# Moving the tail of one expert behind the head of the next in an eight-expert layer

## The reference, cut to what matters

```
disp[e, slot] = x[token]                       # up to 384 slots for each expert
h = np.maximum(np.einsum('ecd,edf->ecf', disp, w1), 0.0)    # 384 -> 1024
y = np.einsum('ecf,efd->ecd', h, w2)                        # 1024 -> 384
out[token] = gate_w[token] * y[expert_idx[token], pos[token]]
```

## Time and profile before

| | |
|---|---|
| median of 3 runs | 415.0 us (414.7 to 415.39) |
| the profiled execution, its own time | 415.56 us |
| its span, first to last instruction | 413.7 us |
| granted TensorE clock, mean | 0.997 |
| PE busy | 406.2 us, 98% |
| DVE, ACT, POOL busy | 242.4, 188.1, 231.4 us |
| chain of work that ended last | PE 88%, DVE 4%, issue 3%, DMA 3% |

### The profile page before, as it was taken

The page is one execution under the profiler, slowest core; times in us unless marked ns, Lnnn a source line. Parts: engine busy times, 40 slices in busy tenths (PEclk is TensorE's granted clock), DMA queues, the critical chain, the costliest instruction groups (busy, mean ns, idle before and its releaser), DMA issues.

```text
span 413.7 us, 9445 instructions
## 1 busy us (share of the span) xinstructions
PE 406.2 (98%) x3697; PEld 390.3 (94%) x3697; DVE 242.4 (59%) x576; ACT 188.1 (45%) x409; POOL 231.4 (56%) x239
## 2 busy tenths in 40 slices
PE   8999999999999999999999999999999999999995
PEld 8799799999999999999999999999999999999995
DVE  7787955376576547654663487785635546364522
ACT  4786553233333333333343455552645455474420
POOL 3789865567856685668234336065083562826531
PEclk9999999999999999999999999999999999999998
DMA  7998997214030403020018001827383845729000
GB/s 281 399 395 341 348 371 255 72 49 150 10 119 2 139 21 118 2 87 21 2 19 345 2 2 38 326 77 238 135 304 99 346 147 217 279 100 363 8 31 28
DMA packets 18650, 64.98 MB, mean 157 GB/s; under 512 B 2203, under 2 KB 11717, under 8 KB 16432
## 3 DMA queue, kind: packets, MB, share of 16 engines
q1 hardware_dynamic: 16672, 59.67, 39.5%
q0 software_dynamic: 1792, 4.73, 3.0%
q10 hardware_dynamic: 144, 0.00, 0.0%
HBM read 51.98 MB, written 13.21 MB: 158 GB/s over the span
## 4 chain that ended last, share of the span: by engine, by line
PE 88%; DVE 4%; issue 3%; DMA 3%; POOL 1%; ACT 1%; POOLq 0%; SPq 0%; DVEq 0%
PE bank L1369 26%; PE bank L1371 25%; PE bank L1370 24%; PE bank L1390 2%; DMA xrow<-slots 2%; PE bank L1419 1%; PE bank L1455 1%; PE bank L1459 1%; PE bank L1693 1%; PE bank L1448 1%; PE bank L1451 1%; PE bank L1546 1%; PE bank L1728 1%; PE bank L1729 1%; PE bank L1632 1%
## 5 line engine op out<-in xcount | busy, mean ns | idle before, releaser
L707 POOL TENSOR_TENSOR g_lo<-elu,g_hi 128x256 fp32r<-128x256 f32 x95 | 73.7, 777 | 86.9 <-ACT g_hi L882 86.6
L1369 PE MATMUL bank<-xt,wd_hi 128*128 128x256 f32 x285 | 80.5, 283 | 0.6 <-DVE elu L1197 0.6
L1371 PE MATMUL bank<-xt,wd_lo 128*128 128x256 f32 x285 | 80.4, 282 | 0.0
L1370 PE MATMUL bank<-xt,wd_hi 128*128 128x256 f32 x285 | 80.3, 282 | 0.0
L873 ACT ACTIVATE elu<-elu 128x256 f32<-128x256 f32 x96 | 40.1, 418 | 76.4 <-DVE elu L1189 75.9
L1369 PE MATMUL bank<-wd_hi,g_hi 128*128 128x392 f32 (+1 forms) x192 | 67.4, 351 | 0.0
L1371 PE MATMUL bank<-wd_hi,g_lo 128*128 128x392 f32 (+1 forms) x192 | 65.2, 340 | 0.0
L1370 PE MATMUL bank<-wd_lo,g_hi 128*128 128x392 f32 (+1 forms) x192 | 65.1, 339 | 0.0
L1197 DVE SCALAR_TENSOR_TENSOR elu<-elu,bank 128x256 f32<-128x256 f32 x96 | 40.3, 419 | 41.1 <-ACT elu L873 41.1
L882 ACT CAST g_hi<-elu 128x256 fp32r<-128x256 f32 x96 | 39.0, 406 | 44.1 <-DVE elu L1197 44.1
L1369 PEld LDWEIGHTS bank<-xt,wd_hi 128*128 128x128 f32 x285 | 53.9, 189 | 1.2 <-DVE elu L1197 1.1
(11 more groups left out here) (220 smaller groups left out, 943.7 us busy)
## 6 DMA issues: line engine op xcount, KB each, us to landing
we_raw<-wexp SPq DMA_DIRECT2D x8, 1536.0 KB, 6.5
wd_raw<-wexp SPq DMA_DIRECT2D x8, 1536.0 KB, 7.4
rkt<-rkt SPq DMA_DIRECT2D x12, 512.0 KB, 5.7
nat<-nat SPq DMA_DIRECT2D x9, 672.0 KB, 5.4
xrow<-slots SPq DMA_DIRECT2D x16, 193.0 KB, 7.4
wd_raw<-win SPq DMA_DIRECT2D x4, 768.0 KB, 8.6
wd_raw<-wout SPq DMA_DIRECT2D x4, 768.0 KB, 9.0
wo_tr<-wouttr SPq DMA_DIRECT2D x1, 3072.0 KB, 17.6
```

Source lines behind the costliest of these rows:

```text
L707: nc.gpsimd.tensor_tensor(g_lo[:, f % 4, :], elu[:, f % 2, :], g_hi[:, f % 4, :].bitcast(F32), ALU.subtract).then_inc(s_glo, 1)
L1369: mm(dst, w_hi, x_hi, start=start, stop=False)
L1370: mm(dst, w_hi, x_lo, start=False, stop=False)
L1371: return mm(dst, w_lo, x_hi, start=False, stop=stop)
```

## The change

On TensorE, second-layer groups 6 and 7 of an expert move behind first-layer groups 0 and 1 of the next expert. VectorE's scaling of an expert moves with them, into the next expert behind its `ge_lo` of group 1 (`expert_out`). Second-layer group 0 now waits for the two tiles of `yrow` one by one, and for the w2 pieces one by one as it needs them.

For this the gate values are copied out of `xrow` into a buffer `gate`, just ahead of the token numbers. The rows are then free once these two copies are done. So SP loads the next rows of that buffer ahead of both weight loads, after `s_tok` and no longer after `s_ye`.

```diff
             with sp.Fori(0, NE // 2 - 1) as i:
                 for r in range(2):
+                    sp.wait_ge(s_tok[r], i + 1)
+                    load_x(2 * i + 2 + r, r)
                     sp.wait_ge(s_he, ET * (2 * i + r + 1))
                     load_w(2 * i + 2 + r, r)
                     sp.wait_ge(s_fc2e, ET * (2 * i + r + 1))
                     load_w2(2 * i + 2 + r, r)
-                    sp.wait_ge(s_ye[r], 2 * (i + 1))
-                    sp.wait_ge(s_tok[r], i + 1)
-                    load_x(2 * i + 2 + r, r)
...
             def tokens_of(t, s):
                 dve.wait_ge(s_xr[0], 16 * (t + 1))
+                V.tensor_copy(gate[0][:, t, :], xrow[0][:, t, GATE:GATE + 1])
                 V.tensor_copy(tok_i[0][:, t, :], xrow[0][:, t, TOKEN:XR]).then_inc(s, 1)
...
+            def expert_out(i, r):
+                dve.wait_ge(s_tok[r], i + 1)
+                for t in range(2):
+                    if t == 0:
+                        dve.wait_ge(s_y0, 2 * i + r + 1)
+                    else:
+                        dve.wait_ge(s_fc2e, ET * (2 * i + r + 1))
+                    V.tensor_scalar(yrow[r][:, t, :], ps_ye[t][:, 0:DM], gate[r][:, t, :], None, ALU.mult).then_inc(s_ye[r], 1)
...
+                    if f == 1 and behind:
+                        expert_out(bi, br)
...
                     if f == 5:
                         dve.wait_ge(s_xr[r], 32 * (i + 1))
                         wait_if(dve, s_sout[r], 32 * i)
+                        V.tensor_copy(gate[r][:, :, :], xrow[r][:, :, GATE:GATE + 1])
                         V.tensor_copy(tok_i[r][:, :, :], xrow[r][:, :, TOKEN:XR]).then_inc(s_tok[r], 1)
...
+            def w2_chunk(f):
+                return -(-(f + 1) * DM // ECH)
+
             def fc2_expert(i, r, f, tiles=(0, 1)):
                 pe.wait_ge(s_gelo, ET * (2 * i + r) + f + 1)
-                if f == 0:
-                    pe.wait_ge(s_ehi[r], 2 * N1 * (i + 1))
-                    wait_if(pe, s_elo2[r], N1 * (i + r))
-                    y_before, n_before = other(s_ye, r, i)
-                    wait_if(pe, y_before, 2 * n_before)
+                if w2_chunk(f) > w2_chunk(f - 1):
+                    pe.wait_ge(s_ehi[r], 2 * N1 * (i + 1) - N1 + w2_chunk(f))
+                    wait_if(pe, s_elo2[r], N1 * (i + r) - N1 + w2_chunk(f))
                 cols = slice(W1 + f * DM, W1 + (f + 1) * DM)
                 for t in tiles:
+                    if f == 0:
+                        y_before, n_before = other(s_ye, r, i)
+                        pe.wait_ge(y_before, 2 * n_before - 1 + t)
...
-                    wait_if(pe, s_gelo, q if f == 0 else q - 1)
+                    wait_if(pe, s_gelo, q - 1)
...
+                    if f < 2 and behind:
+                        fc2_expert(bi, br, ET - 2 + f)
                     if more and f >= 2:
                         fc2_expert(i, r, f - 2)
...
-            expert(0, 1, True)
+            expert(0, 1, True, False)
             with pe.Fori(1, NE // 2 - 1) as i:
-                expert(i, 0, True)
-                expert(i, 1, True)
-            expert(NE // 2 - 1, 0, True)
-            expert(NE // 2 - 1, 1, False)
+                expert(i, 0, True, True)
+                expert(i, 1, True, True)
+            expert(NE // 2 - 1, 0, True, True)
+            expert(NE // 2 - 1, 1, False, True)
```

More of the change, by code:

```diff
@@ L134, in expert_rows @@
                 new(f"xe_lo{r}", [128, KT, SN], F32R), new(f"yrow{r}", [128, 2, DM]),
-                new(f"tok_i{r}", [128, 2, 1], U32))
+                new(f"tok_i{r}", [128, 2, 1], U32), new(f"gate{r}", [128, 2, 1]))
     wo_at = top[0]
@@ L143, in build @@
     ge_lo = new("ge_lo", [128, 4, SN], F32R)
-    xrow, xe_hi, xe_lo, yrow, tok_i = zip(rows0, expert_rows(1))
+    xrow, xe_hi, xe_lo, yrow, tok_i, gate = zip(rows0, expert_rows(1))
     wo_tr, end_g = put("wo_tr", [128, KT, DFF], F32, wo_at)
@@ L1257, in tokens_of @@
                 dve.wait_ge(s_xr[0], 16 * (t + 1))
+                V.tensor_copy(gate[0][:, t, :], xrow[0][:, t, GATE:GATE + 1])
                 V.tensor_copy(tok_i[0][:, t, :], xrow[0][:, t, TOKEN:XR]).then_inc(s, 1)
             def gated(t, y):
-                V.tensor_scalar(yrow[0][:, t, :], y, xrow[0][:, t, GATE:GATE + 1], None, ALU.mult).then_inc(s_ye[0], 1)
+                V.tensor_scalar(yrow[0][:, t, :], y, gate[0][:, t, :], None, ALU.mult).then_inc(s_ye[0], 1)
             x2_rows(NB - 1)
@@ L1287, in _ @@
             dve.wait_ge(s_y0, 1)
+            dve.wait_ge(s_atok, 1)
             gated(0, ps_y[0][:, 0:DM])
@@ L1294, in expert_x, with expert @@
                                     xe_hi[r][:, dst[0]:dst[1], :].bitcast(F32), ALU.subtract).then_inc(s_xelo[r], 1)
-            def expert(i, r, more):
+            def expert_out(i, r):
[6 more added lines that the diff above has]
+                    V.tensor_scalar(yrow[r][:, t, :], ps_ye[t][:, 0:DM], gate[r][:, t, :], None, ALU.mult).then_inc(s_ye[r], 1)
+            def expert(i, r, more, behind):
                 ni, nr = (i, 1) if r == 0 else (i + 1, 0)
+                bi, br = (i - 1, 1) if r == 0 else (i, 0)
                 for f in range(ET):
@@ L1314, in expert @@
                         wait_if(dve, s_sout[r], 32 * i)
+                        V.tensor_copy(gate[r][:, :, :], xrow[r][:, :, GATE:GATE + 1])
                         V.tensor_copy(tok_i[r][:, :, :], xrow[r][:, :, TOKEN:XR]).then_inc(s_tok[r], 1)
[L1316 to L1322, removed]
+                if not more:
+                    expert_out(i, r)
             tile_row(s_he, ET, s_lrow)
@@ L1335, in _ @@
             dve.wait_ge(s_fc2e, ET)
+            dve.wait_ge(s_tok[0], 1)
             gated(1, ps_y[0][:, 0:DM])
-            expert(0, 1, True)
+            expert(0, 1, True, False)
             with dve.Fori(1, NE // 2 - 1) as i:
-                expert(i, 0, True)
-                expert(i, 1, True)
-            expert(NE // 2 - 1, 0, True)
-            expert(NE // 2 - 1, 1, False)
+                expert(i, 0, True, True)
+                expert(i, 1, True, True)
+            expert(NE // 2 - 1, 0, True, True)
+            expert(NE // 2 - 1, 1, False, True)
             dve.wait_ge(s_over, 1)
```

## The result

The changed kernel takes 416.09 us (median of 13 runs, 415.21 to 419.86) against 415.22 (13 runs, 414.67 to 415.44) for the kernel before, run beside it: ratio 1.0035, 95% interval 1.0020 to 1.0049. It is slower by 0.35%, more than the 0.2% that can be told from no change, where 414.1 was forecast; 416.09 lies outside the range of 413.5 to 415.4. Two of the 13 executions, 418.33 and 419.86, had a lower mean granted clock (0.995 and 0.989). The profiled execution took 416.33 us, 0.77 more than that of before.

The account below looks back on a forecast made before the run. TensorE's instruction stream was taken to bound the kernel, so only idle slots could be gained. -0.90 (boundary stalls) - 0.20 (rows) + 0.20 (late w1) = -0.9 us: 415.0 becomes 414.1, range for 8 in 10 413.5 to 415.4.

Parts of the forecast that it names:

- The term of +0.2: First pass: w1 of expert 2 leaves 5.1 us later, lands after 7.2 us, costing +0.2 us, bounds 0 and +1.9.
- The slack: First pass: w1 may land until 292.57 before group 5 of expert 1 is delayed; each us beyond costs one.
- rival 2: First pass: w1 behind the early rows lands after 9.0 us at 294.4, +1.9 instead of +0.2, 415.8; chance 0.07.
- The bound of +1.9: Upper bound of the first-pass w1 term, for a landing after 9.0 us instead of 7.2.
- Order on TensorE, -0.90: Six expert boundaries: the 0.15 us stall at new group 2 goes, -0.90 us; more frequent alternating costs nothing.
- Banks of the second layer (rival 4): Scalings into `yrow` hidden with 0.3 us slack; rival: 0.3 to 0.45 us later, 0.15 returns as wait, 415.0; chance 0.08.
- Rows, -0.20 (-0.40 profiled): Rows loaded ahead of the weights land before their transposes, removing 0.40 us profiled; half, -0.2, taken for the median.
- w2, covered: Second weight load leaves later, lands within 14.3 us of w1's issue; cast due at 15.1, covered by 0.8 at worst.
- Lock-out at 273.9 (rival 1, 0.20): Gate copy delays VectorE's second w1 piece; GpSimd might go first, `hrow` starts at 281.4, +1.2 us, 415.3; chance 0.20.
- Gate copy behind GpSimd (rival 3, 0.03): Group 5 of every expert: gate copy locked out behind GpSimd's split, new group 0 waits, 6 x 1.0, 420; chance 0.03.

Follow-up runs that it names:

- late_w1_rows_behind: Changed kernel, but in the first pass SP waits for the token copy, then issues w1, w2, rows; 414.18 us, ratio 0.9977 to the kernel before.
- half_rows: Changed kernel, but in the first pass half the columns of both row tiles go ahead of w1, the other half behind; 414.76 us, ratio 0.9998.
- one_tile_ahead: Changed kernel, but in the first pass one of two row tiles goes ahead of w1, the other behind; 414.37 us, ratio 0.9983.
- rows_early_only: Changed kernel with gate copies and early rows kept, but the old orders of TensorE and VectorE; 417.21 us, ratio 1.0063.
- w2_apart: Changed kernel, but in the first pass the w2 load waits until w1 has landed; 416.35 us, ratio 1.0017.
- rows_landed_w2_apart: Changed kernel, but in the first pass w1 waits until the rows have landed, and w2 until w1 has landed; 418.26 us, one run.
- rows_landed_first: Changed kernel, but in the first pass w1 is issued only when the rows have landed; 418.17 us, ratio 1.0077.
- experiment 4: The run `w2_apart`: changed kernel with w2 held until w1 has landed in the first pass; 416.35 us, ratio 1.0017.
- experiment 3: The run `late_w1_rows_behind`: changed kernel with the token wait in front but rows last in the first pass; 414.18 us, ratio 0.9977.
- 4 and 6: `w2_apart`, and three first passes: `rows_landed_first`, `rows_landed_w2_apart`, and w1 alone, with rows and w2 held until it landed (414.11 us, one run).
- w1_first: Changed kernel, but in the first pass alone w1 of expert 2 is issued ahead of its rows again; 414.48 us, ratio 0.9978.
- rows_between: Changed kernel, but with the rows between the two weight loads in every pass (w1, rows, w2); 414.5 us, ratio 0.9976.
- rows_last: Changed kernel with its new TensorE order, but rows behind both weight loads in every pass; 418.55 us, ratio 1.0090.
- w1_in_two: Changed kernel, rows still ahead, but each w1 loaded as two transfers, the first third with its own semaphore; 415.55 us, ratio 0.9997.

## Why the prediction was wrong

**The step that failed** is the first pass: "I take 7.2, nearer to the 6.1 of a load alone than to the longest landing of 9.0". The term of +0.2 measured +2.0. Everything around that number held. w1 was to leave at "about 285.4": 285.51. The slack was to end with a landing at 292.57, each us beyond costing one us, once: the cast at 294.49 is 1.92 beyond, and the loss was 1.90 and a refill of 0.10. Counted from the last matmul ahead of the gap (here 294.26, so the limit lies 1.69 before it), the rule holds within 0.02 us in each run:

| run | w1 issued | cast starts | limit | beyond | gap measured |
|---|---|---|---|---|---|
| `late_w1_rows_behind` | 283.94 | 290.32 | - | none | none |
| `half_rows` | 284.73 | 291.48 | - | none | none |
| `one_tile_ahead` | 284.87 | 292.62 | 292.55 | 0.07 | 0.05 |
| `rows_early_only` | 285.78 | 294.58 | 292.86 | 1.72 | 1.70 |
| changed kernel | 285.51 | 294.49 | 292.57 | 1.92 | 1.90 |
| `w2_apart` | 285.42 | 294.66 | 292.69 | 1.97 | 1.95 |
| `rows_landed_w2_apart` | 287.63 | 294.88 | 292.49 | 2.39 | 2.38 |
| `rows_landed_first` | 287.55 | 295.09 | 292.41 | 2.68 | 2.66 |

What happened is rival 2, "Early rows, late w1", priced at 415.8 with a chance of 0.07. Its argument for it was wrong (w2 right behind, experiment 4), and so was the argument against it: "only rows and no weights stand in front of it". They are what stretches the landing (experiment 3; 4 and 6 for its tail). The bound of +1.9 was in the text, but it was left out of the range; with it the sum gave 414.1 + 1.7 = 415.8, near the 416.09 measured.

The other steps, in their order:

- **Order on TensorE, -0.90:** right, 17.45 per expert, and 0.90 between `rows_early_only` and the changed kernel. No pitch was lost to the alternation.
- **Banks of the second layer (rival 4):** no wait of TensorE for `yrow`. The scalings start at 324.99, and with 1.13 for the pair the first ends near 325.6, ahead of the matmul at 326.13.
- **Rows, -0.20 (-0.40 profiled):** right in kind, no transpose waits for rows in the changed kernel. The median of 0.20 is not separable from the spread of runs.
- **w2, covered:** right, its cast in group 5 never waits.
- **Lock-out at 273.9 (rival 1, 0.20):** did not happen. `hrow` starts at 280.21, against 280.15 in the earlier trace rows:

```profile
272.67 0.14 DVE L1257 COPY gate<-xrow 128x1 f32<-128x1 f32 x1
272.74 0.14 DVE L1258 CAST tok_i<-xrow 128x1 uint32<-128x1 f32 x1
272.80 2.35 DVE L1285 TENSOR_TENSOR wd_lo<-wd_raw,wd_hi 128x1024 fp32r<-128x1024 f32 x2
...
280.21 0.69 DVE L1248 TENSOR_SCALAR hrow<-bank 128x512 f32<-128x512 f32 x1 [1.19 <-PE bank L1381]
```

  VectorE's first two pieces took 2.35 us together, undisturbed, as forecast. GpSimd's split starts at 273.94; with the 1.13 us from piece to piece of the earlier trace rows, VectorE's second piece started near 273.93. The margin was three hundredths on paper and one by this, so the order held, but it is not safe.
- **Gate copy behind GpSimd (rival 3, 0.03):** did not happen. The copy took 0.16 at 318.43, GpSimd's split starts at 318.77, 0.34 later; a copy that came second was not tried.

**Settled:** the loss is one stall of 2.0 us in the first pass, it comes with the two row tiles ahead of w1 in that pass, and without them there (`w1_first`, `rows_between`, `late_w1_rows_behind`) the change gives 0.22 to 0.24%. **Open:** why a last engine falls behind when rows are in front, how this grows with their size, whether rows close behind do harm too, and why w1 takes 7.2 us even after they have landed. The profile doesn't say which engine a packet ran on.

## What to carry to other kernels

Ahead of a load on which an in-order engine stands, a small load is not small: price its landing from the longest one in the trace, and when that price decides the sign, put it in the range. A reordering that is right in a loop's steady state has to be costed in its first pass by itself, where the events that pace it come in another order. Give a queue the order of its due times: here w1, then rows, then w2, used in every pass, beat the kernel before by 0.24%, while rows first lost 0.35% and rows last 0.90%.

## What the runs showed of the hardware that was not expected

- Two row loads of 193 KB each ahead of a load of 1.5 MB on the same queue lengthened its landing from 6.4 to 9.0 us in the first pass; in the later passes it was 7.3 to 8.3 in place of 6.2 to 7.7. By an estimate from bytes alone, 386 of 1536 KB are a quarter of 6.4, or 1.6 us. `w2_apart` shows a tail besides: in its last two us 1.9 and then 0.9 of 16 engines still worked for this queue.
- With row loads issued 0.5 to 0.6 us behind it, the load took 7.9 and 7.7 us in two of five later passes (`rows_between`), in place of 6.6 and 6.1 (`rows_last`), and at most 6.8 in the other three. As the kernel before has one 7.7 without them, this is a hint and no more.
- Splitting a load did not bring its end forward: in `w1_in_two` one third landed after 6.2 us, the other two thirds some 10 us after their issue.
- In `rows_landed_w2_apart` TensorE's clock fell behind a gap of 2.38 us, though not in the profiled executions with the gap of 2.66 in `rows_landed_first` or the 1.90 of the changed kernel. Its windows:

```profile
298.50:300.50 2.00, 2.00 (x9) 1.90 (x8) 2.00 (x3) 0.38 (x1) 0.00 (x0) 0.50 0.89 381
300.50:302.50 2.00, 2.00 (x18) 2.00 (x17) 0.79 (x2) 1.17 (x3) 0.00 (x0) 1.00 0.00 0
```

And a matmul of this stretch:

```profile
298.85 0.52 PE L1392 MATMUL bank<-wd_lo,ge_hi 128*128 128x384 f32 x1
```

  From 297.07 to 300.45 the granted clock was 0.50, 1.2 in place of 2.4 GHz, and a 384-column matmul cost 0.32 in place of 0.17 us. Seven matmuls of 256 columns and six of 384 took 3.38 us there in place of 1.87 (7 x 0.117 and 6 x 0.174), 1.5 us on top of the gap itself. The three other executions of `rows_landed_first` took 1.0 to 1.6 us more than its profiled one, at a mean clock of 0.995 to 0.996 in place of 0.999. That fits the same fall, since 3.4 us at half clock take 0.004 off the mean of 415 us, but no profile shows it. So a stall can cost more than its own length.
